# Attention and two MLPs on one core: the third weight matrix kept item by item, more of the second MLP prepared before the last projection

## The reference

```python
# attention with a threshold: 4 batches, 8 heads, 576 tokens, 64 wide
scores = scale * np.matmul(q, k.transpose(0, 1, 3, 2))
scores = np.where(scores >= max(scores) - tau, scores, -1e9)
attn = softmax(scores); x = attn @ v            # -> x: 2304 tokens x 512
# first MLP (w_in 512x1024, w_out 1024x512)
h = x @ w_in
solu = h * softmax(h)
ln = (solu - mean) / np.sqrt(var + 1e-06) * g_ln
x = ln @ w_out
# second MLP (w_in 512x2048, w_out 2048x512)
h = x @ w_in
g = np.maximum(h, 0.0) + np.log1p(np.exp(-np.abs(h)))
out = g @ w_out                                  # 2304 x 512
```

## Time and profile before

| | us |
|---|---|
| median of 3 runs (900.02 to 900.76) | 900.24 |
| the profiled execution, its own time | 898.82 |
| its span, first to last instruction | 897.1 |
| PE busy in the span | 865.2 |
| DVE, ACT, POOL busy | 634.2, 566.3, 331.4 |

### The profile page before, as it was taken

The page is one execution under the profiler, slowest core; times in us unless marked ns, Lnnn a source line. Parts: engine busy times, 40 slices in busy tenths (PEclk is TensorE's granted clock), DMA queues, the critical chain, the costliest instruction groups (busy, mean ns, idle before and its releaser), DMA issues.

```text
span 897.1 us, 16879 instructions
## 1 busy us (share of the span) xinstructions
PE 865.2 (96%) x6248; PEld 718.7 (80%) x6248; DVE 634.2 (71%) x1286; ACT 566.3 (63%) x1040; POOL 331.4 (37%) x425
## 2 busy tenths in 40 slices
PE   6799999999989999999999899999999999999998
PEld 4566666666667889898899798999899899899896
DVE  4999999999955633614431999767767767767765
ACT  2778898787866533424442876667667667667664
POOL 2555677555534601102110433323323323323322
PEclk9999999999999999999999999999999999999999
DMA  6623413343000100000001710000000000000000
GB/s 169 176 68 81 109 43 83 90 106 114 10 1 13 36 1 1 2 1 1 1 12 31 252 36 1 35 1 1 36 1 1 36 1 1 35 0 0 35 0 35
DMA packets 30394, 37.16 MB, mean 41 GB/s; under 512 B 4720, under 2 KB 18544, under 8 KB 30320
## 3 DMA queue, kind: packets, MB, share of 16 engines
q1 hardware_dynamic: 29920, 35.90, 14.3%
q10 hardware_dynamic: 400, 0.30, 0.1%
HBM read 31.46 MB, written 4.72 MB: 40 GB/s over the span
## 4 chain that ended last, share of the span: by engine, by line
PE 38%; issue 21%; POOL 10%; ACT 1%; DVE 1%; POOLq 0%; ACTq 0%
PE h_ps L943 12%; PE y_ps L1076 11%; POOL w_lo L487 10%; PE f_ps L1136 7%; PE m_ps L1052 6%; PE lt_ps L1088 1%; PE o_ps L1014 1%; ACT p_sb L551 0%; DVE ln_lo L809 0%; DVE g_lo L888 0%; ACT ln_hi L588 0%; POOLq L486 0%; DVE g_hi L886 0%; ACT u L679 0%; ACT w_hi L511 0%
## 5 line engine op out<-in xcount | busy, mean ns | idle before, releaser
L487 POOL TENSOR_TENSOR w_lo<-w_raw,w_hi 128x512 fp32r<-128x512 f32 x96 | 135.0, 1406 | 298.6 <-ACT w_hi L663 298.4
L540 ACT ACTIVATE expd<-s_ps,ntop 128x576 f32<-128x576 f32 x144 | 105.6, 741 | 55.4 <-DVE ntop L749 55.4
L663 ACT CAST w_hi<-w_raw 128x512 fp32r<-128x512 f32 x96 | 59.7, 622 | 119.2 <-PE f_ps L1136 118.2
L872 DVE SCALAR_TENSOR_TENSOR g<-u,z 128x384 f32<-128x384 f32 x96 | 63.3, 660 | 95.7 <-ACT u L679 95.7
L1052 PE MATMUL m_ps<-y_hi,w_lo 128*128 128x384 f32 x384 | 131.0, 341 | 0.0
L1052 PE MATMUL m_ps<-y_lo,w_hi 128*128 128x384 f32 x384 | 129.8, 338 | 0.0
L1052 PE MATMUL m_ps<-y_hi,w_hi 128*128 128x384 f32 x384 | 128.5, 335 | 0.0
L1136 PE MATMUL f_ps<-w_hi,g_hi 128*128 128x512 f32 x288 | 114.2, 396 | 4.0 <-DVE g_lo L888 3.2
L749 DVE TENSOR_REDUCE ntop<-s_ps 128x1 f32<-128x576 f32 x144 | 106.8, 757 | 14.1 <-PE s_ps L974 9.9
L765 DVE SCALAR_TENSOR_TENSOR kept<-s_ps,thresh,expd 128x576 f32<-128x576 f32 x144 | 112.1, 816 | 6.6 <-POOL thresh L426 3.5
L974 PE MATMUL s_ps<-k_sb,q_sb 64*128 64x288 f32 x512 | 96.5, 460 | 18.2 <-DVE kept L765 17.4
(11 more groups left out here) (88 smaller groups left out, 1744.9 us busy)
## 6 DMA issues: line engine op xcount, KB each, us to landing
q_sb<-q_t SPq DMA_DIRECT2D x28, 288.0 KB, 5.0
v_sb<-v_main SPq DMA_DIRECT2D x16, 256.0 KB, 3.2
stage<-w_in SPq DMA_DIRECT2D x16, 256.0 KB, 2.8
w_raw<-w_out SPq DMA_DIRECT2D x8, 512.0 KB, 5.6
out<-o_sb SPq DMA_DIRECT2D x5, 768.0 KB, 3.5
k_sb<-k_t SPq DMA_DIRECT2D x21, 144.0 KB, 4.6
stage<-w_in SPq DMA_DIRECT2D x4, 512.0 KB, 7.8
stage<-w_out SPq DMA_DIRECT2D x4, 512.0 KB, 6.5
```

What stands on the lines that cost most here:

```text
L487: nc.gpsimd.tensor_tensor(w4[1][:, n % 2, :], w4_raw[:, n % F2, :], f32(w4[0][:, n % 2, :]), ALU.subtract).then_inc(w4lo_made, 1)
L540: nc.scalar.activation(expd[:, tile % 2, :].rearrange("p (a b) -> p a b", a=2), s_ps[tile % 2][:, :, 0:HALF], ACT.Exp, bias=ntop[:, tile % ...
```

## The change

Memory is laid out anew for the second MLP: the third matrix is kept in 16 tensors of one item each (high and low half side by side) in place of two large ones, and the items are put where memory is dead early (items 1, 2 and 11 where the first MLP's `x_hi`, `x_lo` and `ln` lay, 0 in a gap, 3 to 10 over the first matrix, 12 to 15 over `ln_hi`, `ln_lo` and the second matrix). The first two blocks of rows of the fourth matrix get a buffer of their own that nothing else uses (`w4_first`), loaded during the first MLP; the statistics of the first MLP become one tensor.

The order changes so: EARLY is 4, `up` of blocks 0 and 1 come after `project` of group 4, then the transpose of tile 17, a wait for the low part of tile 16, and `up` of blocks 2 and 3, all before `project` of group 5. ACT casts items 0 to 7 between its copies of group 4 and behind them, takes `soft` of block 0 before the high part of tile 17 and `soft` of 1, 2 and 3 with the casts of items 8 to 11 and of two blocks of the fourth matrix during the last projection; DVE follows. SP loads items as buffers become free, without the wait for the last projection, and the seven other loads of the fourth matrix come behind all of them, when that projection ends.

```diff
-AHEAD = 4
-EARLY = 2
+EARLY = 4
+PREPARED = 12
...
+        w4_first = sb("w4_first", [P, 2, DM])
...
-        w3_lo = sb("w3_lo", [P, C, DFF2], FP32R, where=phase)
...
+        def w3_item(n):
+
+            w3_items[n] = sb(f"w3_{n}", [P, 2, C, P], FP32R, where=phase)
...
+        w3_item(1)
+        w3_item(2)
+        w3_item(11)
+        g_hi = sb("g_hi", [P, GR, GC], FP32R, where=phase)
...
+        w3 = [[item[:, half, :, :] for item in w3_items] for half in range(2)]
...
             for n in range(STAGES, W_ITEMS):
 
                 sp.wait_ge(w_lo, parts(n - STAGES + 1))
                 sp.dma_start(staged(n)[0], staged_source(n)).then_inc(stage_in[n % STAGES], 16)
-                if n >= W_ITEMS - F2 + STAGES:
-                    m = n - (W_ITEMS - F2 + STAGES)
-                    if m == 0:
-
-                        sp.wait_ge(y_made, C * MG)
-                    if m < F2 // 2:
-
-                        wait(sp, w4_in[m % W4_LOADS], 16 * (m // W4_LOADS))
-                        sp.dma_start(w4_raw[:, 2 * m:2 * m + 2, :],
...
+                if n == W3:
+                    load_w4(0)
+
+            sp.wait_ge(y_made, C * MG)
+            for m in range(1, F2 // 2):
+                load_w4(m)
...
-                            if isinstance(group, int) and group == MG - 2 and m == 1:
-
-
-                                act.wait_ge(h_made, MT)
-                                act.wait_ge(ln_made, MT)
-                                act.wait_ge(lt_made, MT - 1)
-                                for j in range(EARLY):
-                                    w_high(C + F1 // 2 + j)
-                                y_high(0, 0)
+                            if isinstance(group, int) and group == MG - 2:
+                                first_w3(m)
+                            if isinstance(group, int) and group == MG - 1:
+                                next_w3(m)
...
+            def first_w3(m):
+
+                if m == 0:
+                    act.wait_ge(h_made, MT)
+                    for n in range(3):
+                        w_high(W3 + n)
+                if m == 1:
+                    y_high(0, 0)
+                    w_high(W3 + 3)
+                if m == 2:
+                    for n in range(4, 7):
+                        w_high(W3 + n)
+
+            def next_w3(m):
+
+                if m == 0:
+                    w_high(W3 + 9)
+                    soft(3, 3)
+                if m == 1:
+                    w_high(W3 + 10)
+                if m == 2:
+
+                    act.wait_ge(lt_made, MT - 1)
+                    w_high(W3 + 11)
...
-            for n in range(4):
+            for n in range(3):
                 mlp1(MT // 6, n)
+            w_high(W3 + 7)
 
             act.wait_ge(ones_made, 6)
-            act.wait_ge(lt_made, MT)
-            for j in range(EARLY, AHEAD):
-                w_high(C + F1 // 2 + j)
+            act.wait_ge(ln_made, MT)
+            soft(0, 0)
+            mlp1(MT // 6, 3)
+            soft(1, 1)
+            w4_high(0, 0)
+            w4_high(1, 1)
+            w_high(W3 + 8)
+            soft(2, 2)
             mlp1(MT // 6, 4)
...
+            w4_high(2, 2)
+            w4_high(3, 3)
+
+            for j in range(EARLY, F2):
+                if j - EARLY + PREPARED < F2:
+                    w_high(W3 + j - EARLY + PREPARED)
                 soft(j, j)
-                m = j // 2
-                act.wait_ge(w4_in[m % W4_LOADS], 16 * (m // W4_LOADS + 1))
                 w4_high(j, j)
...
-                    for m in range(EARLY):
+                    for m in range(7):
+                        if m == 3:
+                            y_low(0, 0)
                         w3_low(m)
-                    y_low(0, 0)
                 if after_product(i, n):
                     transposed_low(i, n - 2)
+                if isinstance(i, int) and tile == MT:
+                    w3_low(7)
...
-                if isinstance(i, int) and i == 0 and n + AHEAD < F2:
+                if isinstance(i, int) and i == 0 and n in (1, 3):
                     def between():
-                        w3_low(n + AHEAD)
+                        w3_low(8 + n // 2)
+                if isinstance(i, int) and i == 0 and EARLY <= n < EARLY + F2 - PREPARED:
+                    def between():
+                        w3_low(n - EARLY + PREPARED)
+                if isinstance(i, int) and i == 0 and n == EARLY:
+                    for m in (10, 11):
+                        w3_low(m)
...
-                    j = tile - (MT - 2)
-                    if j == 1:
+                    if tile == MT - 2:
+                        first_up(0)
+                        first_up(1)
+                    else:
 
                         pe.wait_ge(ltlo_made, MT - 2)
                         transpose_row(tile, n % 2)
-                    first_up(j)
+
+                        pe.wait_ge(ltlo_made, MT - 1)
+                        first_up(2)
+                        first_up(3)
...
-                        pe.wait_ge(y_out, C * MG)
+                        pe.wait_ge(y_out, C * MG - 1)
```

More of the change, by code:

```diff
@@ L147, in build @@
         names = "top ntop esum esum_e inv ssum nmean sq msq var rstd"
-        st = {n: sb("st_" + n, [P, 2], where=phase) for n in names.split()}
-        first_words = 2 * 2 * C * P + 6 * DFF1 + 2 * len(st)
+        st_all = sb("st", [P, 32], where=phase)
+        st = {n: st_all[:, 2 * k:2 * k + 2] for k, n in enumerate(names.split())}
+        first_words = 2 * 2 * C * P + 6 * DFF1 + 32
         sb("gap1", [P, SCORE_WORDS - first_words], where=phase)
@@ L294, in staged, with w4_rows @@
             src = stage[:, n % STAGES, 0:C * P].rearrange("p (a n) -> p a n", a=C)
-            return src, w3[0][:, :, m:m + P], w3[1][:, :, m:m + P]
+            return src, w3[0][m // P], w3[1][m // P]
+        W3 = C + F1 // 2
+        def w4_rows(n, count):
+            return w4_first[:, n:n + count, :] if n < 2 else w4_rest[:, n - 2:n - 2 + count, :]
         def parts(n):
@@ L362, in _, with load_w4 @@
                     load_values(pair)
+            def load_w4(m):
+                wait(sp, w4_in[m % W4_LOADS], 16 * (m // W4_LOADS))
+                sp.dma_start(w4_rows(2 * m, 2), w4_d[2 * m * P:(2 * m + 2) * P, :].rearrange("(a p) n -> p a n", p=P)
+                             ).then_inc(w4_in[m % W4_LOADS], 16)
             for n in range(STAGES, W_ITEMS):
@@ L638, in y_high @@
                                ).then_inc(yhi_made, 1)
[L640 to L650, removed]
-            for n in range(4):
-                mlp1(MT // 6, n)
-            act.wait_ge(ones_made, 6)
-            act.wait_ge(lt_made, MT)
-            for j in range(EARLY, AHEAD):
-                w_high(C + F1 // 2 + j)
-            mlp1(MT // 6, 4)
             def w4_high(j, n):
                 wait(act, f_made, j - 1)
-                nc.scalar.copy(w4[0][:, n % 2, :], w4_raw[:, n % F2, :]).then_inc(w4hi_made, 1)
+                if isinstance(j, int) and j < F2:
+                    act.wait_ge(w4_in[j // 2 % W4_LOADS], 16 * (j // 2 // W4_LOADS + 1))
+                nc.scalar.copy(w4[0][n % 2], w4_rows(n % F2, 1)[:, 0, :]).then_inc(w4hi_made, 1)
             def exponential(j, n):
@@ L692, in soft @@
                 logarithm(j, n)
-            for j in range(F2):
-                if j + AHEAD < F2:
-                    w_high(C + F1 // 2 + j + AHEAD)
+            def first_w3(m):
[18 more added lines that the diff above has]
+                    w_high(W3 + 11)
+            for n in range(6):
+                mlp1(0, n)
+                if n >= 2:
+                    if n == 2:
+                        act.wait_ge(o_made, SIXES)
+                        act.wait_ge(x_made, SIXES)
+                    w_high(C + n - 2)
+            with act.Fori(1, MT // 6) as i:
+                for n in range(6):
+                    mlp1(i, n)
+            for n in range(3):
+                mlp1(MT // 6, n)
+            w_high(W3 + 7)
+            act.wait_ge(ones_made, 6)
+            act.wait_ge(ln_made, MT)
[6 more added lines that the diff above has]
+            soft(2, 2)
+            mlp1(MT // 6, 4)
+            w4_high(2, 2)
[3 more added lines that the diff above has]
+                    w_high(W3 + j - EARLY + PREPARED)
                 soft(j, j)
-                m = j // 2
-                act.wait_ge(w4_in[m % W4_LOADS], 16 * (m // W4_LOADS + 1))
                 w4_high(j, j)
@@ L903, in outputs @@
                     nc.vector.tensor_copy(o_sb[:, k, :], f_ps[k][:, :]).then_inc(f_out, 1)
-            for m in range(EARLY, AHEAD):
-                w3_low(m)
             def mlp2(i, n):
@@ L1051, in up @@
                     for m, (w, y) in enumerate(((w3[0], y_hi), (w3[0], y_lo), (w3[1], y_hi))):
-                        last = nc.tensor.matmul(m_ps[n % 4][:, 0:GC], w[:, k, (n % F2) * P:(n % F2 + 1) * P],
+                        last = nc.tensor.matmul(m_ps[n % 4][:, 0:GC], w[n % F2][:, k, :],
```

(2 more changed lines are left out.)

32 lines of the change are left out of this document (20 added, 12 removed).

## The result

The changed kernel takes 892.76 us (median of 6 runs, 892.23 to 893.0) against 900.13 us before (6 runs, 899.59 to 900.76): 7.4 us or 0.8% faster, ratio 0.9918 with a 95% interval of 0.9905 to 0.993. The forecast was 895.2 us in a range from 892.8 to 897.6 us: the direction was right, the gain was 7.4 us in place of 5.1, and the median lies just under the range.

The account below looks back on a forecast made before the run. PE, busy 96% of the span, was taken to bound the kernel; closing its waits, 0.71 + 0.33 + 2.99 + 0.31 + 0.73 = 5.07 us, was to take 900.24 to 895.2 us, range 892.8 to 897.6 us.

Parts of the forecast that it names:

- the five gaps: PE's waits from the last but one projection into the second MLP's first group, all to close: 5.07 us.
- A: Before the transpose of tile 17, PE waits for the low part of tile 15: excess 0.71 us.
- B: Before the last projection, PE waits for the low part of tile 17: 0.22 us, 0.33 us with the restart.
- C: Before `down` of block 0, PE waits for `g_lo` of block 0: 2.88 us, 2.99 us with the restart.
- C's restart: Longer first step of PE after the wait before `down` of block 0: 0.11 us.
- D: Wait of PE at `down` of block 1: excess 0.20 us, 0.31 us with the restart.
- E: At `down` of block 10, PE waits for a `g_lo`: excess 0.62 us, 0.73 us with the restart.
- rival 1: Late fourth-matrix load: blocks 2 and 3 wait for their rows, up to 2.3 us, 897.5 us; chance 0.12.
- The layout: New addresses of the third matrix in `up`: 2.1 us either way seen as possible, nothing taken.
- The second rival: Faster steps in `up` by the new addresses: 2.1 us less, 893.1 us; chance 0.08.
- The sign that the prediction named for it: Mean `m_ps` duration away from 335 to 341 ns would show changed `up` steps.
- Over 3 us of slack: First group: `g_lo` of block 4 at 505.5 or 506.7 us, its `down` at 509.6 us.

Follow-up runs that it names:

- experiment 7: Changed kernel with `soft` of block 1, too, ahead of the high part of tile 17 on ACT: 892.87 us.
- experiment 8: Changed kernel with the load of the fourth matrix's rows 2 and 3 issued fourth and not first when the last projection ends: 894.38 us.
- experiment 1: Kernel before with two pads (32 bytes ahead of the staging buffers, 64 ahead of the third matrix's high half), nothing else: 897.27 us against 899.83.
- experiment 5: Whole computation left out, PE alone on eight buffers filled once, operands at varied start addresses: `up` steps of 173.3 to 177.7 ns.
- experiment 6: Kernel before with 18 dummy 128x128 transposes on PE between `up` of block 3 and the first `down`: 899.61 us against 900.21.
- experiment 9: PE alone, `up` and `down` in turn, 64 combinations of start addresses of activations, g buffers and fourth-matrix slots: periods of 4,151 to 4,214 ns.
- experiment 2: Changed kernel, order untouched, with the two halves of 13 of the 16 items 32 bytes apart modulo 64: 891.82 us.
- number 11: Changed kernel with pads putting all weights, g buffers, slots and activations at multiples of 128 bytes: 893.42 us, changed kernel beside it 892.63 us.

## Why the prediction was right or wrong

**What bounds the kernel, and the five gaps: right for the profiled execution.** PE bounds; up to the first `down` A, B and C gave 3.98 us where 3.92 us were promised, and C's restart, D and E 1.07 us where it was 1.15 us, with DVE's share of that stretch down from 92% to 69%. The projection was to begin at 476.15 us; it began at 476.83 us in a trace that runs 0.73 us late from the start. But D and E stand in traces without the slow stretch, and by the mean clocks those are the rare executions.

**ACT, DVE and SP before and in the last projection: right.** Low part 17 was to come 1.7 us ahead of its need and came 1.85 us ahead; pushed further by one `soft`, it held PE (experiment 7). The load for blocks 2 and 3 was to need 3.9 us and had 5.8; it landed in 3.5 us, and experiment 8 shows what stood behind rival 1, with its price at 1.7 us of wait. The Trainium skill's sentence on interleaving ("DMA: Bandwidth & Descriptors", "Issuing engines are not separate DMA queues") speaks of transfers that different engines start, which no run here has side by side; on the one queue here the order decided, and experiment 8's load was 4.6 us later at the fourth place.

**The layout: wrong, and this is the step that failed.** The prediction saw 1.8 ns between the two sites, allowed 2.1 us either way, and then took nothing, without a reason of its own. The period fell by 21 ns, 1.9 us in all, nearly the bound. The same layout effect alone, in the kernel before, is worth 2.6 us (experiment 1). That placement acts at all speaks against taking the Trainium skill's page "SBUF — State Buffer", section "Who interferes with whom", to mean that operands' addresses are free for PE: its rule is about engines waiting on each other, and with only PE at work (experiment 5) the steps still differed by 2.5%. The second rival had the right mechanism and nearly the right price (893.1 us), with a chance of 0.08. That its time came so near is in part luck, as it left out the clock. The sign that the prediction named for it would have missed it: the mean `m_ps` durations after are 336 and 337 ns, inside the 335 to 341 ns of before, and only the starts show the change. As the sign of the effect could not be read from the rows of before, even odds between it and its opposite, and a range that went past its price, would have been in order. The sentence that the prices of an item's cast and subtraction are set by the count of elements held here (the subtraction takes 0.68 us for 15 items before and for all 16 after), but not in general: in experiment 1's trace the same subtraction takes 1.74 us for nine items. Why is not known.

```profile
506.07 1.73 DVE L818 TENSOR_TENSOR w_lo<-stage,w_hi 128x512 fp32r<-128x512 f32 x1
510.24 1.74 DVE L818 TENSOR_TENSOR w_lo<-stage,w_hi 128x512 fp32r<-128x512 f32 x1
```

**The clock: a term that was missing.** The prediction read "at the full clock" from one profiled execution. By the mean clocks that one was an exception: most executions of the kernel before have a half-clock stretch behind gap C. The changed kernel has no gap there, and no such stretch in its trace. Filled with dummy work the kernel before runs 0.6 us faster (experiment 6, at the edge of its interval). In the profiled pair it is hidden, and the spans differ by 6.2 us only: the profiled execution of before had luck at the start as well, with half as long at 1.2 GHz there (block 0 starts 0.73 us earlier in it).

**The sum.** Against the profiled execution of before, less its luck at the start: 3.98 us up to the first `down`, 1.07 us for C's restart, D and E, 1.9 us for the period, 6.9 us in all; the spans' 6.2 us and the 0.73 us of that luck are the same. Against the usual execution, 1.6 us of slow stretch stand in the place of the 1.07 us: 7.5 us, with 7.4 us measured. The 5.07 us of the prediction were taken over from the one to the other without a look at what sets them apart.

**A small slip.** "Over 3 us of slack" for `down` of block 4 is 509.6 - 506.7 = 2.9 us by the longer of its own two figures; nothing hangs on it.

**What stays open.** Why certain pairs of start addresses cost PE 2 to 4 ns a matmul is not known. Distance modulo 128 bytes orders much of the tables but not all, and the kernel's periods differ from those of experiment 9 by up to 34 ns in 4,190. The order of work alone, on the old placement, was not run: experiment 2 was meant as that and turned out a third placement. No usual execution of the kernel before was traced, so that its slow stretch and its missing D and E are put together from mean clocks and from experiments 1 and 6. Why the same idle of 2.7 us is followed by the lower clock in one execution and not in another is open.

## What to carry to other kernels

A wait on the critical engine costs its length, its restart, and, where the clock falls behind it, the slow stretch, less the later waits that this stretch hides; one profiled execution may not show it, so look at the mean clock of all executions. When a kernel bound by PE has its buffers moved, compare the start-to-start step of the same matmuls before and after, before any gain or loss is put down to the order of work. Where such a kernel is otherwise done, a pad of 32 to 96 bytes ahead of an operand is a cheap trial, to be measured each time: here it was worth 2.6 us of 900 on the kernel before and 1.6 us on the changed one, and another pad (number 11) lost 0.8 us.

## What the runs showed of the hardware that was not expected

- Matmuls of one shape, with all data ready and no other engine at work, start every 173.3 to 177.7 ns (384 columns) and every 230.8 to 233.4 ns (512 columns), by the start addresses of weights and moving operand in steps of 32 bytes. Pairs of `up` and `down` spread over 4,151 to 4,214 ns. In the kernel, two pads took the pair from 4,200 to 4,173 ns.
- An idle stretch of 2.7 us on PE was followed by a granted clock of 1.2 GHz for some 3.4 us in one trace (experiment 1) and by the full clock in another (before). By the mean clocks the first is the usual case. The nine matmuls that followed took 3.71 us in place of 2.16 us.
- Of four loads of 512 KB issued back to back on one queue, the place decided the landing: the data for the same cast was there 4.6 us later when its load went fourth and not first.
